# One more drain on GpSimd, ahead of the last expert's scatters, in a fused attention and two-layer expert kernel

## What is computed

```
state = gamma * state + k v^T ; y = scale * q state        # 4 batches, 8 heads, 768 steps
x = y as (3072, 512)
x = (s * relu(x @ w_in)^2 + b) @ w_out                     # 512 -> 2048 -> 512
order = argsort(-(x @ w_gate).flatten())                   # 8 experts, 384 tokens each
for idx in order: give token idx//8 to expert idx%8, if both are free
for e in range(8):
    out[mask_e] = relu(x[mask_e] @ w1[e]) @ w2[e]          # 512 -> 1024 -> 512
```

## Time and profile before

| | us |
|---|---|
| median of 3 runs | 936.05 |
| lowest and highest | 935.75, 936.5 |
| the profiled execution | 937.1 |
| its span, first to last instruction | 935.3 |
| outside the span in that execution | 1.8 |
| TensorE busy | 924.5 (99% of the span) |
| GpSimd busy | 231.1 (25%) |

### The profile page before, as it was taken

One profiled execution on the slowest core, in us unless ns is written; L12 is line 12 of the kernel. 1 busy time (PEld: TensorE's weight loads), 2 busy tenths in 40 slices (PEclk: granted clock), 3 DMA queues, 4 the chain that ended last, 5 costly groups with the idle time before them and its releaser, 6 DMA issues.

```text
span 935.3 us, 18539 instructions
## 1 busy us (share of the span) xinstructions
PE 924.5 (99%) x7461; PEld 749.0 (80%) x7461; DVE 515.9 (55%) x1218; ACT 296.0 (32%) x557; POOL 231.1 (25%) x216
## 2 busy tenths in 40 slices
PE   8999999999999999999999999999999999999997
PEld 6777777777787777777777777778999999999996
DVE  6775566565666466467676676762534434434420
ACT  3453444343443452010101010101443534534421
POOL 5232222222222000001110111001443552643611
PEclk9999999999999999999999999999999999999999
DMA  9996757666665478667676867284635645645500
GB/s 336 314 317 228 244 215 254 224 232 228 242 232 193 180 248 320 241 208 224 212 235 196 238 200 229 85 271 144 226 114 179 202 122 172 203 135 158 180 34 34
DMA packets 81317, 192.93 MB, mean 206 GB/s; under 512 B 8880, under 2 KB 17584, under 8 KB 81232
## 3 DMA queue, kind: packets, MB, share of 16 engines
q1 hardware_dynamic: 77200, 178.98, 56.9%
q0 software_dynamic: 3840, 12.59, 4.1%
q10 hardware_dynamic: 192, 0.19, 0.1%
HBM read 128.54 MB, written 63.18 MB: 205 GB/s over the span
## 4 chain that ended last, share of the span: by engine, by line
PE 93%; DVE 3%; DMA 2%; SPq 1%; issue 0%; ACT 0%; POOLq 0%; POOL 0%; DVEq 0%
PE bank L1062 28%; PE bank L1183 28%; PE bank L1240 14%; PE bank L1225 14%; PE bank L995 3%; PE bank L905 1%; PE bank L1203 1%; PE bank L929 1%; PE bank L864 1%; PE bank L893 1%; PE bank L1096 1%; DMA staging<-in_w_in 1%; DMA early_qT<-in_q_turned 1%; PE bank L965 0%; SPq L446 0%
## 5 line engine op out<-in xcount | busy, mean ns | idle before, releaser
L1062 PE MATMUL bank<-x,wi_hi 128*128 128x512 f32 x768 | 240.7, 395 | 0.0
L1062 PEld LDWEIGHTS bank<-x,wi_hi 128*128 128x128 f32 x768 | 141.7, 188 | 44.6 <-issue 10.9
L689 POOL TENSOR_TENSOR w_lo<-w_raw,w_hi 128x512 fp32r<-128x512 f32 x72 | 93.9, 1312 | 302.0 <-ACT w_hi L803 301.8
L1062 PE MATMUL bank<-x,wi_lo 128*128 128x512 f32 x384 | 149.6, 390 | 0.0
L1183 PE MATMUL bank<-wo_b,g_back 128*128 128x512 f32 x552 | 137.6, 399 | 0.0
L1311 DVE SCALAR_TENSOR_TENSOR u_sb<-u_sb,cst 128x512 f32<-128x512 f32 x96 | 77.9, 812 | 98.5 <-ACT u_sb L733 98.5
L803 ACT ACTIVATE w_hi<-w_raw 128x512 fp32r<-128x512 f32 x128 | 76.5, 636 | 158.1 <-DMA w_raw<-in_w 157.8
L733 ACT ACTIVATE u_sb<-bank 128x512 f32<-128x512 f32 x96 | 57.4, 598 | 184.1 <-PE bank L1062 182.0
L1183 PEld LDWEIGHTS bank<-wo_b,g_back 128*128 128x128 f32 x552 | 99.7, 189 | 19.0 <-issue 0.8
L1617 DVE TENSOR_TENSOR w_lo<-w_raw,w_hi 128x512 fp32r<-128x512 f32 x56 | 62.6, 1118 | 62.4 <-ACT w_hi L803 62.3
L1612 DVE SCALAR_TENSOR_TENSOR e_lo<-bank,e_hi 128x384 fp32r<-128x384 f32 x64 | 35.5, 554 | 99.7 <-ACT e_hi L841 99.7
(11 more groups left out here) (209 smaller groups left out, 1214.5 us busy)
## 6 DMA issues: line engine op xcount, KB each, us to landing
g_rows<-g_sb SPq DMA_DIRECT2D x96, 512.0 KB, 3.0
g_back<-g_rows SPq DMA_DIRECT2D x80, 512.0 KB, 4.0
w_raw<-in_w SPq DMA_DIRECT2D x128, 256.0 KB, 3.8
x_rows<-x SPq DMA_DIRECT2D x25, 256.0 KB, 5.0
g_back<-g_rows SPq DMA_DIRECT2D x16, 384.0 KB, 4.6
kT<-in_k_turned SPq DMA_DIRECT2D x22, 256.0 KB, 4.0
qT<-in_q_turned SPq DMA_DIRECT2D x22, 256.0 KB, 3.7
vin<-in_v SPq DMA_DIRECT2D x22, 256.0 KB, 4.1
```

The lines of the kernel that those rows point to most:

```text
L689: pool.tensor_tensor(low, w_raw[:, (p * E_PIECES + n) % RAW, :], high.bitcast(F32), ALU.subtract).then_inc(w1_lo_done, 1)
L1062: last = pe.matmul(up[i % 2][:, :], w[:, t, fs], x[:, half, t, :], start=(t == 0 and n_ == 0), stop=(t == DT - 1 and n_ == 2))
```

## The change

Behind the loop over the experts, GpSimd gets one instruction more, a drain. It stands behind expert 6's scatters (the seventh expert's) and ahead of the first wait of expert 7's. It raises no semaphore and nothing waits for it but what stands behind it on GpSimd. No other engine's list changes, and the order of GpSimd's other instructions is the same.

More of the change, by code:

```diff
@@ L707, in _ @@
                         split_low(p + 1, n)
+            pool.drain()
             scatter(EXPERTS - 1)
```

## The result

| | before | changed |
|---|---|---|
| median of 16 runs, us | 936.07 | 934.02 |
| lowest and highest, us | 935.11, 937.18 | 933.33, 934.91 |
| span of the profiled execution, us | 935.3 | 932.5 |

The ratio is 0.9979 with a 95% interval of 0.9973 to 0.9986: 2.05 us less between the medians. The forecast was 934.15, the gain 1.9 us.

What follows compares the result with a forecast made beforehand. GpSimd's final drain was taken to end the span, 1.96 us after SyncE. New drain 0.0, final drain minus 1.9: 936.05 to 934.15 us; likeliest case 933.8 to 934.5, 8-in-10 range 933.8 to 936.3.

Steps and rivals of the forecast that it cites:

- (a): Final drain goes through all DMAs since the last drain, 0.083 us each; 3 left instead of 48; chance 0.62.
- fixed tail: First rival: final drain's tail doesn't depend on the number of DMAs; time stays 936.05 us; chance 0.25 including no effect.
- The 960 ns: Gathers' issue time, compared with 0.94 us for the last, as a sign that issuing gets neither dearer nor cheaper.
- the first two are cleared while the third is in flight: Final drain, last three scatters: third cleared 0.083 us after its landing, so the drain ends at 932.9 to 933.0.
- Nothing on the path: Added drain ahead of the last three scatters: its 3.7 us, ending at 906.6, hidden by GpSimd's idle time before 927.39.
- The upper bound, 911.9: Added drain's latest end: 901.85 plus slowest landing 5.1 plus 4.9 us for 45 DMAs, 15.5 us before 927.39.
- the sign that the forecast named: In the changed profile, the added drain starts at about 901.7 to 901.9 and takes some 4 to 5 us.
- the 0.2% bound: Differences up to 0.2% (1.87 us) can hardly be told from no change; the 1.9 us gain lies on it.
- Mixture: Second rival: final drain has a fixed part and a part by number, ends at 934.0; time 934.95; chance 0.08.
- Slower by late landings: Third rival: last three scatters land late after a drain, up to 2.4 us; time 936.55 or 938.45; chance 0.05.
- does not do what it says: Added drain is dropped or counts only arithmetic; comes out as the first rival, 936.05 us.

Runs made afterwards that it cites:

- the runs with 6 to 24 DMAs: Kernel before with drains at ends of expert-loop turns instead; one after the first turn: 935.32 us against 935.89, ratio 0.9997; the others timed once.

## Why the prediction was right, and where it was not

**What ends the span.** Right: GpSimd's final drain, 1.96 us behind SyncE. It shrank to under SyncE's arrival, and SyncE was next, as forecast. The final drain was forecast to shrink "from 5.20 us to about 3.1"; it takes 3.13.

**The choice of (a).** Right, over a fixed tail, which the result refutes, and over a cost paid once, which the forecast hadn't named and the runs with 6 to 24 DMAs exclude. The argument was from one row, and a fixed tail had been left 0.25. The 960 ns that the forecast calls the median of the first two gathers is the median of all three; nothing hangs on it. The straight line of 0.58, 1.06, 1.54 and 2.05 us is what the row itself couldn't give.

**The price for a DMA.** 0.083 us was forecast, 0.08 measured with everything landed. For a final drain with transfers in flight the step "the first two are cleared while the third is in flight" was wrong in kind: half of the work for every DMA, the old ones too, comes only behind the last landing. In the sum this made no difference, since 3 x 0.04 us after the landing stays under SyncE's arrival. To that extent the number is luck of the place: the final drain had only 3 DMAs left, and there the wrong order of work and the right one give the same time. With more left they don't: for 12 DMAs 1.9 us was expected and 2.29 came, for 24 it was 2.0 and 2.78.

**The new drain.** "Nothing on the path" was right. Its end was forecast at 906.6, on the time of the kernel before (3.7 us after the descriptor work); it came 5.39 us after it. The step that failed is the same one: the third scatter's landing took 4.5 us (4.6 in the kernel before, so no doing of the drain) and the second pass waited for it. The upper bound, 911.9, held. The trace shows it starting at 899.1, earlier than the forecast 901.7, while the scatters ahead of it are still at work: its duration counts from its issue, and reads some 2.8 us longer than its work behind them. So the sign that the forecast named, 4 to 5 us, was missed with 8.2.

**The size.** 1.9 us forecast, 1.98 between the tails in the trace and 2.05 between the medians. The gain lay on the 0.2% bound as said: 0.21% by the ratio, with an interval of 0.14 to 0.27% that has the bound inside it.

**The rivals.** Fixed tail: refuted. Mixture: its fixed part of 1.1 us behind the landing isn't there; with one DMA the drain ends 0.08 us behind it. What is true of it is that half of the time by number comes only behind the landing. Slower by late landings: the three last scatters land 2.7 us after their start as before. What a drain does cost the DMA behind it is a restart, 0.73 us in place of 0.30 to 0.39, and it was hidden here by the wait for the products. That the drain "does not do what it says": refuted by the result, and its own record is 8.2 us long.

The Trainium skill's page "PSUM — Partial Sum Buffer", section "Engine vs sequencer instructions", has a drain wait until the engine is fully idle. By these traces that is short of what GpSimd's drain does: behind its own DMAs it waits for their landing (1707 ns with two in flight), and ends only 0.04 us for each DMA later (1.88 us with 45).

No version faster than the changed kernel came of this. Its final drain already ends 0.1 us ahead of SyncE, whose wait for the landing of the last scatter is set by TensorE's last product, the copy and the transfer.

## What to carry to other kernels

Look at what comes behind the last instruction of the kernel's own text: here a drain of the framework was the last to arrive, and the profile's busy times, the chain and the waits hardly show it. Where GpSimd has issued many DMAs, by the runs of this one kernel, a drain of its own in a stretch where it is idle anyway moves their 0.08 us each out of the tail; place it as late as the cover allows, but ahead of the last DMAs, since a drain between them waits for a landing. Count the gain only to the next arrival: of the 3.7 us that were taken out of the final drain's work, 2.0 reached the time.

## What the runs showed of the hardware

- A drain on GpSimd takes 0.1 us plus 0.08 us for each DMA that GpSimd issued since its last drain, all of them landed (0.58 us for 6, 3.99 for 48). With no DMA since the last drain it takes 41 ns.
- With a DMA in flight it doesn't end before the landing, and half of the time for each DMA (0.041 us) follows behind that: 1.88 us for 45, 1.02 for 24.
- The number counts, not the size: 24 transfers of 128 bytes add 2.0 us to the tail.
- A DMA that has nothing else to wait for starts 0.73 us after the drain ahead of it, in place of 0.30 us after another DMA.
- The transfers that SyncE issues don't count: the drain at 681 us has several hundred of them before it and takes 0.58 us for GpSimd's six.

What the two passes are, and which unit makes them, no run here shows; that they are two is inferred from the slope that doubles and from the landings above.
